# Where two operand sums of the first superblock are made: beside pairs 12 and 14 of the attention stage, or behind its last probabilities

## The reference

```
scores = scale * q @ k.T;  scores = where(0 <= i - j < 64, scores, -1e9)
attn = exp(scores - max);  attn /= sum + 1e-9;  out = attn @ v     # 4 x 8 heads, 576 x 64
x = out.transpose(0, 2, 1, 3).reshape(2304, 512)
P = exp(x @ w_gate - max);  8 times: P /= row sums; P /= column sums; P *= N / E
for e in range(8): out += P[:, e:e+1] * (maximum(x @ w1[e], 0) @ w2[e])   # 512 -> 1024 -> 512
```

## Time and profile before

| quantity | value |
|---|---|
| median of 3 executions | 1604.66 us (1604.3 to 1604.78) |
| the profiled execution's own time | 1606.06 us |
| its span, first to last instruction | 1604.2 us |
| PE busy | 1583.3 us (99%) |
| POOL busy | 990.4 us (62%) |
| DVE busy | 694.2 us (43%) |
| ACT busy | 544.8 us (34%) |

### The profile page before, as it was taken

One profiled execution on the slowest core, in us unless ns is written; L12 is line 12 of the kernel. 1 busy time (PEld: TensorE's weight loads), 2 busy tenths in 40 slices (PEclk: granted clock), 3 DMA queues, 4 the chain that ended last, 5 costly groups with the idle time before them and its releaser, 6 DMA issues.

```text
span 1604.2 us, 24055 instructions
## 1 busy us (share of the span) xinstructions
PE 1583.3 (99%) x8886; PEld 1420.8 (89%) x8886; DVE 694.2 (43%) x1261; ACT 544.8 (34%) x785; POOL 990.4 (62%) x642
## 2 busy tenths in 40 slices
PE   7899999999999999999999999999999999999999
PEld 6789888989899888989989898998989889898988
DVE  6744543443443434434434434434344344344343
ACT  4643242323333342333323233333323333332331
POOL 4985656556565976656565565878556565655652
PEclk9999999999999999999999999999999999999999
DMA  7621212121211213121121212113121212212111
GB/s 218 177 73 67 79 54 79 53 79 52 78 62 69 78 52 119 53 79 61 70 78 52 78 52 78 60 71 118 53 79 53 78 57 73 78 52 78 52 65 39
DMA packets 34159, 120.44 MB, mean 75 GB/s; under 512 B 3904, under 2 KB 4160, under 8 KB 34112
## 3 DMA queue, kind: packets, MB, share of 16 engines
q1 hardware_dynamic: 34112, 119.80, 21.9%
HBM read 115.06 MB, written 4.72 MB: 75 GB/s over the span
## 4 chain that ended last, share of the span: by engine, by line
PE 94%; POOL 4%; issue 1%; DVE 1%; ACT 0%; POOLq 0%; DVEq 0%
PE ps L488 17%; PE ps L487 17%; PE ps L486 16%; PE ps L449 14%; PE ps L445 14%; PE ps L447 14%; POOL probs L833 2%; POOL sc L825 1%; PE ps L343 0%; POOL t_raw L814 0%; PE ps L531 0%; PE ps L355 0%; POOL w_lo L791 0%; DVE x_raw L990 0%; PE ps L366 0%
## 5 line engine op out<-in xcount | busy, mean ns | idle before, releaser
L791 POOL TENSOR_TENSOR w_lo<-w_raw,w_hi 128x1792 fp32r<-128x1792 f32 (+2 forms) x97 | 386.5, 3985 | 540.2 <-ACT w_hi L571 540.2
L626 ACT ACTIVATE h_hi<-ps 128x384 fp32r<-128x384 f32 x384 | 186.5, 492 | 872.3 <-DVE ps L974 434.0
L488 PE MATMUL ps<-w_hi,h_lo 128*128 128x512 f32 x1152 | 454.1, 394 | 0.0
L487 PE MATMUL ps<-w_lo,h_hi 128*128 128x512 f32 x1152 | 453.1, 393 | 0.0
L486 PE MATMUL ps<-w_hi,h_hi 128*128 128x512 f32 x1152 | 451.5, 392 | 0.0
L449 PE MATMUL ps<-xv_hi,w_lo 128*128 128x384 f32 x1330 | 445.8, 335 | 0.0
L445 PE MATMUL ps<-xv_hi,w_hi 128*128 128x384 f32 x1330 | 444.8, 334 | 0.7 <-DVE h_lo L948 0.7
L447 PE MATMUL ps<-xv_lo,w_hi 128*128 128x384 f32 x1330 | 444.3, 334 | 0.0
L948 DVE SCALAR_TENSOR_TENSOR h_lo<-ps,h_hi 128x384 fp32r<-128x384 f32 x384 | 205.9, 556 | 266.8 <-ACT h_hi L626 257.9
L445 PEld LDWEIGHTS ps<-xv_hi,w_hi 128*128 128x128 f32 x1330 | 249.7, 188 | 17.9 <-DVE h_lo L948 2.0
L447 PEld LDWEIGHTS ps<-xv_lo,w_hi 128*128 128x128 f32 x1330 | 249.7, 188 | 16.7
(11 more groups left out here) (87 smaller groups left out, 961.4 us busy)
## 6 DMA issues: line engine op xcount, KB each, us to landing
w_raw<-w SPq DMA_DIRECT2D x192, 512.0 KB, 3.9
qk_buf<-qk SPq DMA_DIRECT2D x16, 576.0 KB, 6.4
v_win<-v SPq DMA_DIRECT2D x16, 288.0 KB, 4.3
out<-x_raw SPq DMA_DIRECT2D x18, 256.0 KB, 4.3
const_sb<-consts SPq DMA_DIRECT2D x1, 176.0 KB, 3.6
wg<-w_gate SPq DMA_DIRECT2D x1, 64.0 KB, 5.1
```

Of the source, the lines that this page charges most:

```text
L487: nc.tensor.matmul(ps_y[t], h_hi[slot][:, f, c], w2_lo[slot][:, f, :], start=False, stop=False)
L488: last = nc.tensor.matmul(ps_y[t], h_lo[slot][:, f, c], w2_hi[slot][:, f, :], start=False, stop=closes)
L626: nc.scalar.activation(h_hi[slot][:, f, half * HT:(half + 1) * HT], o, ACT.Relu)\
L791: last = nc.gpsimd.tensor_tensor(w1_lo[:, slot, c], w1_raw[:, slot, (lo + 1) * BLK:(hi + 1) * BLK], w1_hi[:, slot, c].bitcast(F32), ALU.su ...
```

## The change

Three sections of the program move, and nothing is added or left out. On POOL the sums T2 and T3 leave the pairs 12 and 14 and stand behind weigh(15); the last part of w1's low part moves up from pair 13 to pair 12. On ACT the splits of P6, P7 and P5 stand together behind plain_relu(1), ahead of x_copy(14); P6's stood in iteration 14, P7's behind it, P5's ahead of v_shift(15).

```
@@ ACT, -710,17 +710,16 @@
-                if p == 14:
-                    x_split(0, P6)
-            x_split(0, P7)
             v_shift(NP - 2)
             x_copy(NP - 3)
             exp(NP - 1)
             plain_relu(0)
             w2_split(16, 0, 0)
-            x_split(0, P5)
             v_shift(NP - 1)
             plain_relu(1)
+            x_split(0, P6)
+            x_split(0, P7)
+            x_split(0, P5)
             x_copy(NP - 2)
             x_split(0, P4)
             plain_relu(2)
@@ POOL, -854,12 +853,10 @@
                 if p == 12:
-                    x_sum(0, T2)
-                if p == 13:
                     w1_rest(1, 1, 4, 7)
-                if p == 14:
-                    x_sum(0, T3)
             weigh(NP - 1)
+            x_sum(0, T2)
+            x_sum(0, T3)
             x_rest(0, P6, 1)
             w2_rest(0, 0)
             x_sum(0, T4)
```

## The result

The changed kernel takes 1609.07 us (median of 9 executions, 1607.2 to 1610.52) against 1604.66 us, a ratio of 1.0027 with a 95% interval of 1.0018 to 1.0037: slower by 4.4 us, where 3.4 were forecast. Two more jobs gave 1608.98 against 1604.74 and 1608.71 against 1604.5, so the loss is 4.2 to 4.4 us each time.

The account below looks back on a forecast made before the run. PE carries 94% of the chain, POOL 4% ahead of the windows, through T4 to the gate. T2 and T3 add 3.58 us, weigh(15) gives back 0.17: 1604.66 + 3.41 = 1608.1 us, range 1606.9 to 1609.2.

Parts of the forecast that it names:

- The chain through T4 to the gate: On POOL, ACT and PE: the gate waits for x_copy(15) behind P4's split, which needs T4; gate 3.41 us later.
- The price of T2 and T3: On POOL between weigh(15) and T4: two subtractions of 1.79 us add 3.58 us, at most 3.68.
- What weigh(15) gains: On POOL: weigh(15) starts only 0.17 us earlier, bounds 0 and 0.3, since exp(15) stands behind v_shift(14) and x_copy(13).
- The new wait of mix(15): On PE: mix(15) waits for x_copy(14), starting at about 98.9 instead of 97.28 us, at no cost by itself.
- Nothing else came late behind the gate: Rival behind the gate: something else late, a rest or a load, costs 1 us more; 3 in 100.
- The sum: Up to the gate: 3.58 - 0.17 = 3.41 us later, so 1608.1 us; its own range 1607.7 to 1608.6.
- PE's clock: Rival on PE: its clock falls to 1.2 GHz after two new gaps, losing 2 to 2.6 us, 1610.7; 6 in 100.
- the evidence that I set against it: On PE: scores(2) behind a 2.01 us gap took 2.08 us, as long as later scores, so that gap didn't slow PE.
- Slower by over 0.2%: Whole kernel: a loss beyond the 3.2 us that a measurement can tell from no change; some 0.74.
- rival of a partial gain: Rival at weigh(15): exp(15) less bound by v's DMA, gain from 0.37 us on, 1604.7 to 1607.8 us; 14 in 100.
- the wider range: Whole kernel: 1606.9 to 1609.2 us, reaching into the partial gain and half a microsecond over the main case.
- Not slower: Rival on POOL: shift(14) to weigh(15) close up, weigh(15) comes 3.58 us earlier or more, down to 1602.6 us; 3 in 100.

Follow-up runs that it names:

- fillers: Changed kernel plus 8 and 10 extra PE products, output never read, in its two new gaps: 1608.01 us; third job 1607.6 us.

## Why the prediction was right, and where it wasn't

**The chain through T4 to the gate: right.** The gate waits for x_copy(15) behind P4's split, and behind the gate nothing changes (1503.2 us in both profiles). With the copies taken out from behind the splits the loss fell from 4.4 to 0.75 us, with T2 and T3 left where the change puts them.

**The price of T2 and T3: right.** 3.58 forecast, 3.60 measured. Their records are 1.82 and 1.85 us at the new place and 1.83 and 1.85 at the old; DVE was busy for 0.56 and 1.36 us of them at the new place and for 1.76 and 1.78 at the old, so less work on DVE made them no shorter. The Trainium skill's "GPSIMD Engine Reference", section "Key points", which tells of contention with some of VectorE's instructions, would have let them be shorter there; this trace shows no such gain.

**What weigh(15) gains: right mechanism, a little undersized.** 0.17 forecast, 0.41 measured from shift(13), outside the bound of 0.3 that I set. It is even beyond the 0.37 from which on the prediction puts the change within 0.2%. v_shift(14) started 0.16 us earlier (11.40 after shift(13), from 11.56), since v landed sooner; x_copy(13) followed it after 0.99 us, where I had taken 1.06 for that step, and its wait of 0.18 was gone. That v's DMA and ACT's order eat the gain was shown by moving exp(15): T2 then starts 2.75 us earlier.

**The new wait of mix(15): right.** 1.63 us, and no cost by itself. Nothing else came late behind the gate; the stall of the maximum only shows once the gate is freed.

**The sum: 3.41 forecast, 3.17 in the profiles, 4.4 in the median.** The term that was missing is PE's clock. I had it as a rival with 6 in 100, and the step that failed is the evidence that I set against it: that scores(2) stood behind 2.01 us of idle time and took 2.08. That was one execution. The same scores behind the same gap took 3.72 in another. The clock doesn't fall always or never behind such a gap; it falls in a share of the executions, so the clock wasn't another case beside the forecast but a part of the mean: 8 of 28 executions at 0.998, none of 22 with fillers, and 1.1 us between the two medians on one chip. The price of the rival was off too: 2 to 2.6 us per fall by the warming products, 1.70 measured at the gate. Executions at 1.000 in both kernels stand 1607.7 - 1604.32 = 3.4 us apart, close to the 3.17 of the chain. The Trainium skill's page "TensorE: Matmul & The Clock Gate", section "HAM oscillation — how this bites in real kernels", tells of matmuls that go at half rate again after each wait, in a kernel that waits some 3 to 5 us for its DMA. Here gaps of 2.0 us were enough, with 1.09 instead of 0.61 us per row of the gate, in one execution and not in the next. Of the 0.999 executions I can't say which had their fall at the start and which at the gate.

**Slower by over 0.2%: in part luck.** The chain alone makes 3.17 us, 0.20%, which is just inside the prediction's own bound of 3.2 us: by the profiles this was its rival of a partial gain. (The executions at 1.000 give 3.4 us, just outside; the bound lies within what the runs can't tell apart.) The falls of the clock carried the median over that bound, and with 1609.07 us out of the 1607.7 to 1608.6 that the sum gave; it lies 0.13 us inside the wider range.

**The rivals.** The partial gain (v landed a little sooner) and the fall of the clock both took place, side by side. Not slower is out for the change as made. What was right in "not slower" is that 5.2 us of POOL's time lay idle; it took two other moves on ACT to use it.

## What to carry to other kernels

Taking work off an engine in a pipelined stage helps only if what releases its next instruction moves too. Here three waits grew by 3.1 us in sum, because exp(15) stood behind a copy that waited for a DMA. Before moving a producer later, look at what stands behind its consumer in the consumer's queue: the gate needed neither T3 nor T4, only a copy that was queued behind their splits. And a new gap on PE can cost more than its length: look at the clock of many executions, since a single profile can catch it up or down.

## What the runs showed of the hardware

In five profiles PE's clock fell, each time within some 1.2 us of the end of an idle time of 1.95 to 2.01 us. In other executions, of the changed kernel among them, it stayed up behind the same idle time. In the profile with exp(15) first it also stayed up at the gate behind 2.23 us. A fall cost 1.70 us over the gate.

Three of the five falls came early, between 10 and 30 us, one of them in a kernel that equals the one before up to there. The 32 of 84 executions of the kernel before that show 0.999, probably by such a fall, are 0.8 us slower in the median than the other 52.

A 128x768 fp32 subtraction on POOL took 1.82 and 1.85 us beside DVE work of 0.56 and 1.36 us, and 1.83 and 1.85 us beside DVE work of 1.76 and 1.78 us.
